# Chunk 0 of a fused attention and gated expert kernel: the last 64 channels of two tokens on the two column halves of TensorE, and one maximum moved

## What is computed

```python
# local attention: every token mixes itself and the 6 tokens before it, a weight per head and tap
w = softmax(weight_gen, axis=-1)                   # 4 x 4160 x 8 heads x 7 taps
out[b, s, h, :] = sum over k of w[b, s, h, k] * x[b, s - 6 + k, h, :]     # 192 channels = 8 x 24
# gated expert on that result
h = relu(out @ w_in)                               # 192 -> 1024
conv = 3 taps over the tokens of h, a weight per channel
result = (h * sigmoid(conv)) @ w_out               # 1024 -> 192
```

## Time and profile before

| | |
|---|---|
| median of 3 runs | 718.46 us (718.26 to 718.46) |
| the profiled execution | 718.5 us, span 716.7 us |
| TensorE busy, matmuls | 706.4 us, 99% |
| VectorE busy | 614.3 us, 86% |
| GpSimd busy | 614.2 us, 86% |
| ScalarE busy | 497.3 us, 69% |
| granted TensorE clock | full throughout |

### The profile page before, as it was taken

The page is one execution under the profiler, slowest core; times in us unless marked ns, Lnnn a source line. Parts: engine busy times, 40 slices in busy tenths (PEclk is TensorE's granted clock), DMA queues, the critical chain, the costliest instruction groups (busy, mean ns, idle before and its releaser), DMA issues.

```text
span 716.7 us, 9863 instructions
## 1 busy us (share of the span) xinstructions
PE 706.4 (99%) x3839; PEld 634.6 (89%) x3839; DVE 614.3 (86%) x549; ACT 497.3 (69%) x636; POOL 614.2 (86%) x285
## 2 busy tenths in 40 slices
PE   8997999999999999999999999999999999999998
PEld 8756889899999999999989898989899999999997
DVE  7998999999988989898898989898999989885630
ACT  3658867696767676776977676677777867676641
POOL 5999999999997999999899999989898899925310
PEclk9999999999999999999999999999999999999999
DMA  8420312103031222212030210203020200000001
GB/s 239 145 104 1 91 51 77 44 22 100 18 100 30 72 60 55 86 36 95 23 101 16 69 50 23 93 23 108 27 93 23 50 21 20 23 18 23 23 29 34
DMA packets 26297, 41.44 MB, mean 58 GB/s; under 512 B 3864, under 2 KB 23678, under 8 KB 24461
## 3 DMA queue, kind: packets, MB, share of 16 engines
q1 hardware_dynamic: 26250, 40.81, 18.7%
HBM read 28.02 MB, written 12.78 MB: 57 GB/s over the span
## 4 chain that ended last, share of the span: by engine, by line
PE 95%; ACT 2%; DVE 2%; issue 0%; DMA 0%; SPq 0%; ACTq 0%
PE out_ps L952 45%; PE z L930 41%; PE turn_ps L974 3%; PE turn_ps L952 2%; PE z L942 1%; PE z L991 1%; PE turn_ps L991 0%; PE out_ps L991 0%; ACT hidden L634 0%; PE z L952 0%; DVE z L773 0%; DVE z L779 0%; ACT gated L653 0%; DMA logits<-in_weight_gen 0%; DVE xb L824 0%
## 5 line engine op out<-in xcount | busy, mean ns | idle before, releaser
L486 POOL TENSOR_TENSOR weighted<-x_win,soft 128x1344 f32<-128x1344 f32 (+1 forms) x128 | 351.1, 2764 | 7.4 <-DMA x_win<-in_x 7.3
L952 PE MATMUL out_ps<-wo,gated 128*128 128x192 f32 x2000 | 346.0, 326 | 0.2
L952 PEld LDWEIGHTS out_ps<-wo,gated 128*128 128x128 f32 x2000 | 326.9, 190 | 8.4 <-ACT out_sb L689 0.8
L603 POOL TENSOR_TENSOR gated<-gated,hidden 128x1022 f32<-128x1022 f32 (+1 forms) x117 | 248.4, 2123 | 73.9 <-ACT gated L653 73.7
L773 DVE SCALAR_TENSOR_TENSOR z<-hidden,cw,z 128x1022 f32<-128x1022 f32 (+1 forms) x134 | 164.6, 1229 | 59.8 <-ACT z L640 59.0
L634 ACT ACTIVATE hidden<-z 128x1024 f32<-128x1024 f32 (+1 forms) x136 | 134.5, 989 | 106.5 <-PE z L930 99.0
L779 DVE SCALAR_TENSOR_TENSOR z<-hidden,cw,z 128x1022 f32<-128x1022 f32 (+1 forms) x134 | 166.2, 1240 | 4.2
L640 ACT ACTIVATE z<-hidden,cw 128x1022 f32<-128x1022 f32 (+1 forms) x134 | 144.9, 1081 | 4.2
L814 DVE TENSOR_REDUCE attn_a<-weighted 128x256 f32<-128x1792 f32 (+1 forms) x62 | 124.8, 2012 | 0.0
L653 ACT ACTIVATE gated<-z 128x1022 f32<-128x1022 f32 (+1 forms) x117 | 115.1, 984 | 12.0 <-PE out_ps L952 7.1
L930 PE MATMUL z<-xa_hi,wa_hi 128*128 128x512 f32 (+1 forms) x264 | 100.1, 458 | 5.4 <-ACT gated L653 5.2
(11 more groups left out here) (83 smaller groups left out, 394.6 us busy)
## 6 DMA issues: line engine op xcount, KB each, us to landing
x_win<-in_x SPq DMA_DIRECT2D x11, 1344.0 KB, 6.4
out<-out_sb SPq DMA_DIRECT2D x111, 96.0 KB
logits<-in_weight_gen SPq DMA_DIRECT2D x12, 224.0 KB
x_win<-in_x SPq DMA_DIRECT2D x2, 1008.0 KB
out<-out_sb SPq DMA_DIRECT2D x16, 84.0 KB
x_win<-in_x SPq DMA_DIRECT2D x1, 1176.0 KB
x_win<-in_x SPq DMA_DIRECT2D x1, 768.0 KB, 10.1
wo<-in_moe_w_out SPq DMA_DIRECT2D x1, 768.0 KB, 13.9
```

The costliest lines, as they stand in the source:

```text
L486: return engine.tensor_tensor(to, rows, s, ALU.mult)
L603: nc.gpsimd.tensor_tensor(gated_flat(c, n), gated_flat(c, n), hidden[:, n % 3, 1:1 + c.size], ALU.mult) \
L952: last = nc.tensor.matmul(bank[0:end - begin, 0:D], gated[:, j, begin:end], wo[:, j, :], start=(j == 0), stop=(j == J - 1))
```

## The change

Tokens 1, 3, 5, 7 keep their seven matmuls for the first 128 channels. Their last 64 channels are summed and turned by a new function, `sum_and_turn_last`, for two tokens at once: token 1 (or 5) writes partitions 0 to 63 of the bank and token 3 (or 7) partitions 64 to 127, one column half of the array each. `turn` does the same with tokens 0 and 2, and 4 and 6, as plain matmuls. Rounds 1 and 3 become the kind "b": two pieces of 64x256 for ScalarE and for VectorE instead of one of 64x512. The maximum of chunk 2 goes into `top` in place of a z bank, its shift on VectorE stands behind the fourth low part, and TensorE waits for two shifts ahead of the second rest.

```diff
-ROUNDS_FIRST = [[("a", 0, 4)], [("single", 0, 4)], [("a", 4, 8)], [("single", 4, 8)]]
+ROUNDS_FIRST = [[("a", 0, 4)], [("b", 0, 4)], [("a", 4, 8)], [("b", 4, 8)]]
...
-            elif kind == "single":
-                found.append((slice(D2, P), slice(first, stop), at, stop - first))
-                at += stop - first
             else:
-                found.append((slice(0, D2), slice(first, first + c.half), at, c.half))
-                found.append((slice(D2, P), slice(first + c.half, stop), at, c.half))
-                at += c.half
+                half = (stop - first) // 2
+                found.append((slice(0, D2), slice(first, first + half), at, half))
+                found.append((slice(D2, P), slice(first + half, stop), at, half))
+                at += half
...
-            if c in CHUNKS[1:3]:
+            if c is CHUNKS[1]:
                 return z[1][0:c.parts, 0, c.number * TOKENS * H:(c.number + 1) * TOKENS * H]
...
                 low_part(c, 0)
-                shift(CHUNKS[2])
                 low_part(c, 1)
                 low_part(c, 2)
                 low_part(c, 3)
+                shift(CHUNKS[2])
...
-                    for i in range(first, stop) if kind != "b" else range(first // 2, stop // 2):
+                    half = (stop - first) // 2
+                    for i in range(first, stop) if kind == "a" else range(first, first + half):
...
-                            src = attn_first[:, i, 0:P] if kind == "a" else attn_first[:, i, D - P:D]
-                        if c is not FIRST or i not in BY_TENSOR:
+                            src = attn_first[:, i, 0:P]
+                        if c is FIRST and kind == "b" and i not in BY_TENSOR:
+                            for u, rows in ((i, slice(0, D2)), (i + half, slice(D2, P))):
+                                last = nc.tensor.matmul(bank_of(c, r)[rows, at * c.parts:(at + 1) * c.parts], attn_first[:, u, P:D],
+                                                        ident[0:c.parts, 0:c.parts], start=True, stop=True)
+                        elif c is not FIRST or i not in BY_TENSOR:
...
+            def sum_and_turn_last(i):
+
+                c, at, first = FIRST, i % 4, BY_VECTOR.index(i)
+                assert BY_VECTOR[first + 1] == i + 2
+                pe.wait_ge(s_weighted_dve, first + 2)
+                bank = bank_of(c, i // 4 * 2 + 1)
+                if bank is soft_bank:
+                    pe.wait_ge(s_weighted_dve, len(BY_VECTOR))
+                for tap in range(K):
+                    for u, rows in ((0, slice(0, D2)), (1, slice(D2, P))):
+                        taps = gated[0:c.parts, first + u, 0:K * D].rearrange("p (k d) -> p k d", k=K)
+                        nc.tensor.matmul(bank[rows, at * c.parts:(at + 1) * c.parts], taps[:, tap, P:D],
+                                         ident[0:c.parts, 0:c.parts], start=(tap == 0), stop=(tap == K - 1))
...
             sum_and_turn(1)
             sum_and_turn(3)
+            sum_and_turn_last(1)
             turn_conv_weights()
-            for i in BY_TENSOR[2:]:
-                sum_and_turn(i)
+            sum_and_turn(5)
+            sum_and_turn(7)
+            sum_and_turn_last(5)
             turn(FIRST, 0)
             turn(FIRST, 1)
             rest_of_weights(0, wa_hi, stage_a)
             turn(FIRST, 2)
             turn(FIRST, 3)
             pe.wait_ge(s_conv_weights, 1)
-            pe.wait_ge(s_shifted, 3)
+            pe.wait_ge(s_shifted, 2)
             rest_of_weights(1, wb_hi, stage_b)
```

More of the change, by code:

```diff
@@ L979, in sum_and_turn @@
             def sum_and_turn(i):
-                c = FIRST
+                c, at = FIRST, i % 4
                 pe.wait_ge(s_weighted_dve, BY_VECTOR.index(i) + 1)
[L983 to L992, removed]
+                taps = places(c, i, 1)[:, 0].rearrange("p (k d) -> p k d", k=K)
+                for tap in range(K):
+                    nc.tensor.matmul(bank_of(c, i // 4 * 2)[:, at * c.parts:(at + 1) * c.parts], taps[:, tap, 0:P],
+                                     ident[0:c.parts, 0:c.parts], start=(tap == 0), stop=(tap == K - 1))
[6 more added lines that the diff above has]
+                    pe.wait_ge(s_weighted_dve, len(BY_VECTOR))
+                for tap in range(K):
+                    for u, rows in ((0, slice(0, D2)), (1, slice(D2, P))):
+                        taps = gated[0:c.parts, first + u, 0:K * D].rearrange("p (k d) -> p k d", k=K)
+                        nc.tensor.matmul(bank[rows, at * c.parts:(at + 1) * c.parts], taps[:, tap, P:D],
+                                         ident[0:c.parts, 0:c.parts], start=(tap == 0), stop=(tap == K - 1))
             def step(k):
```

## The result

The changed kernel took 721.47 us (median of 5; 721.28 to 722.34) against 718.46 us (718.26 to 718.51) on the same chip: a ratio of 1.0044, 95% interval 1.0033 to 1.0056. The forecast was 718.0. The time lies at the upper end of the stated range, where rival A stood with 721.4, but A's mechanism is not what happened. The profiled execution took 721.5 us (span 719.7), 3.0 us more than the one before.

The account below looks back on a forecast made before the run. TensorE was taken as the bound, with VectorE equally late at 42 us. Starting step 0's product 1.77 us earlier, less 1.3 for the moved maximum, left 0.47: 718.5 - 0.5 = 718.0 us, range 717.2 to 721.5.

Parts of the forecast that it names:

- rival A: TensorE's two column halves do not overlap: 0.114 us a record, step 3's product 2.95 us later, 721.4 us; chance 0.22.
- P0: Start of step 0's product on TensorE: forecast 27.55 us, 1.77 us earlier than 29.32.
- What bounds, and where a shift counts: TensorE, busy 99%, bounds; its shift at 42 us, where VectorE arrives too, reaches the end in full.
- the prediction's own signs of being wrong: Halves at another spacing, step 3's product not waiting for VectorE, or the lead at 42 us not that at 74.
- t: Spacing of TensorE's half-array matmul records: between 0.057 and 0.114 us, taken as 0.057.
- s: Cost of one TensorE change between whole array and halves, six places: 0 to 0.19 us, taken as 0.10.
- S0: Start of the first `rest_of_weights` on TensorE: forecast 21.95 us, against 23.93 before.
- From S0 to P0: Stretch from first `rest_of_weights` to step 0's product, with split casts and subtractions: 5.60 us, against 5.39 before.
- The moved maximum: Chunk 2's shift behind VectorE's fourth low part adds 1.30 us before step 0's gate, taking back 1.3 of 1.77 us.
- forecast case: The main forecast, 718.0 us, or 717.4 to 718.6 with the mode-change cost from 0 to 0.19; chance 0.58.
- what would show it: Signs: 1.6 us per 28 half records, step 0's product at 27.5, a 1.2 us wait at step 3, step 10 at 73.3.
- Rival C: VectorE's line to step 0's gate has slack, the moved maximum costs nothing: 1.77 us earlier, 716.7 us; chance 0.08.

Follow-up runs that it names:

- top_psum: Changed kernel with chunk 2's maximum in a PSUM bank, its shift still behind the fourth low part: 717.57 us, ratio 0.999 to the kernel before.
- halves_in_turn: Changed kernel with all seven taps of one column half first, then all seven of the other, instead of by turns: 725.01 us, ratio 1.0087.
- before_shift_behind: Kernel before, without column halves, with chunk 2's shift behind the fourth low part and its maximum in a PSUM bank: 719.26 us, ratio 1.0013.
- before_top_sbuf: Kernel before with only chunk 2's maximum put in SBUF, its shift staying between the first and second low part: 721.64 us, ratio 1.0041.
- fill_gap: Changed kernel with 13 idle matmuls in TensorE's gap ahead of step 3's product: 720.31 us median, ratio 1.0052 to the kernel before.
- shift_front: Changed kernel with chunk 2's shift again between first and second low part, in the z bank, TensorE waiting for three shifts: 717.51 us, ratio 0.9987.

## Why the prediction was wrong

The forecast was 718.0 us and the profiled execution took 721.53. The 3.53 us between them are: P0 0.25 later than forecast, 1.75 more from P0 to step 3 (15.83 and not 14.08), and 1.53 for the clock. That the time fell within the stated range is luck: the range reached so far for a rival that did not happen.

1. *What bounds, and where a shift counts.* Right where the clock stayed full: in top_psum the lead was 1.1 us at both 41.0 and 72.7. In the changed kernel the shift at step 3, 1.53 us, was not the shift at step 10, 3.06; this was one of the prediction's own signs of being wrong, and it is step 6 below. From 49.9 us on nothing changed: the 3.06 us there are the 3.06 at step 10 and the 3.0 at the end.
2. *t, the spacing of half records.* Right: 0.060, with one change between array and halves in each run of 28, against 0.057 taken. halves_in_turn shows that the overlap makes it. The rule on weight loads in the Trainium skill (TensorE: Matmul & The Clock Gate, Part 3) that I weighed for rival A is not borne out here, for the two halves use the same rows and do overlap.
3. *s and S0.* Right: 22.11 against 21.95. The 9.34 us from 12.77 to 22.11 are 0.76 more than the prediction's terms without s (5.16 + 60 x 0.057 = 8.58), 0.13 for each of the six changes against 0.10 taken.
4. *From S0 to P0.* Right in size: 5.69 against 5.60; two subtractions took 0.88 as against 0.86.
5. *The moved maximum.* This is the step that failed. Its first part, that VectorE's work to the gate has no slack, was right; the size of the move was 0.9 to 1.2 us and not 1.3 (0.9 in before_shift_behind and top_psum, 1.2 left over in the changed kernel). Its second part priced the shift by the rows of before, 25.14 to 26.44, although the diff changes an operand of it. The change of `top_of` stands in the diff, and I gave the change of memory no cost. The row that I took was of a subtraction with one input in PSUM, and no row of before showed one with both in SBUF beside GpSimd; that called for bounds from both sides, as I had given them for t. Within the 1.30 us the subtraction stood at 0.62 us, and it measured 2.48. With the maximum in PSUM (top_psum) the time was 717.57, within the 717.4 to 718.6 of the forecast case; an earlier input and a cheaper move than forecast both helped it there. The exponential on ScalarE, which was not to wait for the shift, waited 1.35 us for it.
6. *What that wait sets off.* The prediction had a wait of about 1.2 us ahead of step 3 and no term for the clock. Behind waits of 0.90 us (top_psum) and 1.68 us (before_top_sbuf) the clock stayed full. With 3.01 us it did not, which cost 1.53 us more.
7. *The rivals.* A gave the right number by the wrong way: it wanted half records of 0.114 us and P0 at 30.97, and the trace has 0.060 and 27.80. The spacing of the records and the time of P0, both in the list of what would show it, tell the two apart. Rival C, that the moved maximum costs nothing, falls. None of the rivals was the one that happened, a longer instruction on VectorE.

The page SBUF — State Buffer of the Trainium skill, Who interferes with whom, says that a VectorE instruction with two SBUF inputs contends with a GpSimd instruction that reads SBUF, and calls the ports that the two share an exclusive lock. The traces agree: 2.46 to 2.50 us beside a product of GpSimd in three kernels, 0.62 with GpSimd idle, 0.62 with one input in PSUM. From that rule and the products' length a wait of up to one product, 2.7 us, could have been estimated. That estimate does not cover halves_in_turn, where the wait was 4.9 us.

What stays open: why the executions of before_top_sbuf and of fill_gap scatter over 3 us and more, and when a waiting subtraction is passed over. In both kernels the long executions have the lower mean clock (0.995), and one profile shows a wait for two products; a longer wait with a loss of clock behind it would fit, but only one execution of each kernel has a profile.

## What to carry to other kernels

When a diff changes in which memory an operand lies, price that instruction anew, and look at what GpSimd does at that moment; a buffer name in an access helper can matter more than the change in the title. A gain at one engine counts only up to the next place where another engine is equally late: find that place first, and shorten both lines together. And read a wait of TensorE for its length: those of 0.9 and 1.7 us here cost only themselves, one of 3.0 us cost half as much again in clock.

## What was not expected of the hardware

- A VectorE subtraction of 0.62 us with both inputs in SBUF took 2.46, 2.48, 2.50 and 5.53 us beside GpSimd's products; each time it ended some 0.35 us after the recorded end of a product, and in the last case a later product went first.
- fp32 matmuls of 64 weight columns on the two column halves by turns cost 0.060 us a record; one half alone 0.101; the whole array 0.114.
- After 3.0 us without work TensorE's granted clock fell to 0.50 only when it had been working again for 0.9 us, from 44.5 to 47.9 us. In halves_in_turn, with a wait of 2.67 us, it fell within the wait (39.0 to about 42.4 us). So the loss can fall on the work behind a gap.
- The landing of one input moves the changed kernels and not the one before. TensorE now waits for token 3's product (0.49 us at 12.77), whose start lay at 10.61 in top_psum, 10.93 in shift_front and 11.16 in the changed kernel; the executions of these three spread over 1.0 to 1.4 us, those of the kernel before over 0.3 to 0.7. That the one causes the other is inferred.
